# An expert's third tile of rows turned only where it has one, rows loaded from GpSimd's queue, and four low parts of the last weights made later

## What is computed

```python
def _moe2_ref(x, w_gate, w1, w2, capacity):
    logits = x @ w_gate                      # x: 1536 rows of 384, E = 8 experts
    expert_idx = np.argmax(logits, axis=1)
    ...                                      # gate_w: the softmax of the chosen one
    for i in range(N):                       # disp[e]: up to capacity = 384 rows
        e = expert_idx[i]
        if counts[e] < capacity:
            disp[e, counts[e]] = x[i]
...
    h = np.maximum(np.einsum('ecd,edf->ecf', disp, w1), 0.0)   # w1[e]: 384 x 1024
    y = np.einsum('ecf,efd->ecd', h, w2)                       # w2[e]: 1024 x 384
    ...                                      # out[i] = gate_w[i] * y[its expert, its place]
```

## Time and profile before

| | |
|---|---|
| median of 3 runs | 420.84 us (420.67 to 420.88) |
| the profiled execution | 420.92 us |
| its span in the trace | 419.2 us (mean granted clock 0.997) |

### The profile page before, as it was taken

The page is one execution under the profiler, slowest core; times in us unless marked ns, Lnnn a source line. Parts: engine busy times, 40 slices in busy tenths (PEclk is TensorE's granted clock), DMA queues, the critical chain, the costliest instruction groups (busy, mean ns, idle before and its releaser), DMA issues.

```text
span 419.2 us, 9352 instructions
## 1 busy us (share of the span) xinstructions
PE 403.1 (96%) x3194; PEld 387.9 (93%) x3195; DVE 265.4 (63%) x571; ACT 191.4 (46%) x442; POOL 183.6 (44%) x191
## 2 busy tenths in 40 slices
PE   5799999999999999999999999999999999999992
PEld 5698899999999999999999999998999999999972
DVE  6898877664427434264333789582888797735990
ACT  2879955341221212211123333343859595626950
POOL 3999808554222442224435567253503031103252
PEclk9999999999999999999999999999999999999998
DMA  6997027436980000000100245316996694908500
GB/s 236 405 380 248 3 65 215 148 101 230 367 301 0 35 24 0 0 0 19 38 0 0 75 132 155 111 42 223 378 360 176 211 291 142 322 5 258 165 3 27
DMA packets 34329, 61.74 MB, mean 147 GB/s; under 512 B 4798, under 2 KB 27310, under 8 KB 34288
## 3 DMA queue, kind: packets, MB, share of 16 engines
q1 hardware_dynamic: 31280, 55.92, 39.7%
q0 software_dynamic: 3008, 5.29, 3.7%
HBM read 47.92 MB, written 15.18 MB: 151 GB/s over the span
## 4 chain that ended last, share of the span: by engine, by line
PE 86%; DVE 5%; issue 2%; POOL 2%; PEld 1%; ACT 1%; DMA 0%; POOLq 0%; DVEq 0%; PEldq 0%; ACTq 0%
PE bank L1436 24%; PE bank L1397 23%; PE bank L1619 8%; PE bank L1650 5%; PE bank L1670 4%; PE bank L1720 3%; PE bank L1381 3%; PE bank L1345 2%; PE bank L1373 2%; PE bank L1685 2%; PE bank L1537 2%; PE bank L1588 1%; PE bank L1331 1%; PE bank L1547 1%; PE bank L1445 1%
## 5 line engine op out<-in xcount | busy, mean ns | idle before, releaser
L553 POOL TENSOR_TENSOR g_low<-act_full,g_high 128x384 fp32r<-128x384 f32 x63 | 65.1, 1034 | 111.3 <-ACT g_high L697 111.2
L697 ACT ACTIVATE g_high<-act_full 128x384 fp32r<-128x384 f32 x64 | 33.7, 526 | 146.1 <-DVE act_full L1032 133.5
L1397 PE MATMUL bank<-x_split,w_high 128*128 (+1 forms) x384 | 98.6, 337 | 0.2 <-DVE w_low L945 0.2
L1026 DVE TENSOR_SCALAR neg<-bank,alpha_sb 128x384 f32<-128x384 f32 x64 | 39.4, 616 | 89.0 <-PE bank L1397 89.0
L1397 PEld LDWEIGHTS bank<-x_split,w_high 128*128 128x128 f32 x384 | 68.9, 188 | 0.9 <-DVE w_low L945 0.5
L611 POOL DMA_INDIRECT out<-y_out,token x24 | 30.9, 1289 | 86.2 <-ACT y_out L823 83.0
L1436 PE MATMUL bank<-w_high,g_high 128*128 128x384 f32 x189 | 64.5, 341 | 0.0
L1397 PE MATMUL bank<-x_split,w_low 128*128 (+1 forms) x192 | 64.4, 336 | 0.0
L1436 PE MATMUL bank<-w_high,g_low 128*128 128x384 f32 x189 | 63.8, 338 | 0.0
L1436 PE MATMUL bank<-w_low,g_high 128*128 128x384 f32 x189 | 63.8, 338 | 0.0
L1032 DVE SCALAR_TENSOR_TENSOR act_full<-bank,neg 128x384 f32<-128x384 f32 x64 | 35.7, 557 | 2.4
(11 more groups left out here) (171 smaller groups left out, 841.9 us busy)
## 6 DMA issues: line engine op xcount, KB each, us to landing
w_raw<-chunks SPq DMA_DIRECT2D x96, 192.0 KB, 5.9
w_raw<-chunks SPq DMA_DIRECT2D x32, 384.0 KB, 3.8
rk_in<-att_rk SPq DMA_DIRECT2D x12, 704.0 KB, 6.5
routed_rows<-fill SPq DMA_DIRECT2D x1, 5211.0 KB, 18.0
xe<-routed_rows SPq DMA_DIRECT2D x7, 579.0 KB, 5.4
v_in<-att_v SPq DMA_DIRECT2D x12, 200.0 KB, 6.3
out<-fill SPq DMA_DIRECT2D x1, 2304.0 KB, 23.3
x_split<-x_split POOLq DMA_DIRECT2D x18, 48.0 KB, 2.6
```

The source lines that it names most:

```text
L553: pool.tensor_tensor(gl[:, f % 4, :], act_full[:, f % 2, :], gh[:, f % 4, :].bitcast(f32), ALU.subtract).then_inc(s_gl, 1)
L697: act.activation(gh[:, f % 4, :], act_full[:, f % 2, :], ACT.Copy).then_inc(s_gh, 1)
L1026: dve.tensor_scalar(neg[:, f % 2, :], h, 0.0, alpha_sb[:, f:f + 1], ALU.min, ALU.mult)\
L1397: last = mm(bank[f % 4][:, 0:G], a[:, f, w], x[:, kc, bass.ds(g * G, G)], start=kc == 0 and i == 0, stop=kc == KC - 1 and i == 2)
```

## The change

1. The third tile of an expert's rows is no longer turned during the expert before. It is turned at the head of the expert's own three-tile side, with ACT's and DVE's split there too; the products f = 0 and 1 of tile 0's `expert_down` are moved from behind `flip_up(e, 2, ...)` to between the turn and it. New semaphores count these third tiles; experts without one only raise them.
2. The rows of experts 2 to 7 are loaded from GpSimd's queue. `load_xe(e + 2)` stands before expert e's three scatters, behind the wait for the scatters of e - 1, and waits until expert e's third tile is turned (or passed over). SP's queue holds only the weights.
3. Expert 7's low parts of `w2` for f = 4 to 7 move from expert 6's one-tile side into expert 7's, between its `flip_relu` and `flip_low`.

```diff
         def xe_there(engine, e, tiles):
 
-            if e:
-                engine.wait_ge(s_xe[e % 2], (e + 1) // 2 * 16)
+            if e >= 2:
+                engine.wait_ge(s_xep[e % 2], e // 2 * 16)
+            elif e:
+                engine.wait_ge(s_xe, 16)
...
-        TURN = {3: 0, 5: 1, 7: 2}
+        TURN = {3: 0, 5: 1}
...
             def load_xe(e):
-                if e >= 2:
-                    sp.wait_ge(s_te, (e - 2) * GT + 1 if e > 2 else 2)
-                    sp.wait_ge(s_meta, e - 1)
-                elif e:
+                if e:
...
                 for f in range(NFE):
                     load_w1(e, f)
-                load_xe(e)
                 for f in range(NFE):
                     load_w2(e, f)
...
+            def load_xe(e):
+
+                pool.wait_ge(s_te2 if e > 2 else s_te, e - 2 if e > 2 else 2)
+                pool.wait_ge(s_meta, e - 1)
+                pool.dma_start(xe[:, e % 2, :, :],
+                               disp[ER + e * CAP:ER + (e + 1) * CAP, :].rearrange("(i p) n -> p i n", p=P))\
+                    .then_inc(s_xep[e % 2], 16)
+
...
                 for i in Y_ORDER:
+                    if i == Y_ORDER[0] and e + 2 < E:
+                        load_xe(e + 2)
                     y_scatter(e, i, s_out if e < E - 1 else s_last)
...
-            for i in range(1, GT):
-                xe_high(1, i, bank[X_BANK[i]])
+            xe_high(1, 1, bank[X_BANK[1]])
...
+                    xe_high(e, 2, bank[X_BANK[2]])
                     flip_high(e, 2)
...
+                    def last_low2(*fs):
+                        for f in fs:
+                            if e == E - 1:
+                                split_low2(E - 1, f)
+
                     flip_relu(e, 0, 0)
...
+                    last_low2(4, 5)
                     flip_relu(e, 0, 1)
                     last_low1(3)
+                    last_low2(6)
                     flip_low(e, 0, 0)
+                    last_low2(7)
...
                     if e < E - 1:
-                        for i in range(1, GT):
-                            xe_low(e + 1, i, bank[X_BANK[i]])
+                        xe_low(e + 1, 1, bank[X_BANK[1]])
+                    dve.sem_inc(s_tel2, 1)
                     last_low1(6, 7)
                     if e == E - 2:
-                        low2(0)
-                    low2(1, 2, 3, 4, 5, 6, 7)
+                        low2(0, 1, 2, 3)
+                    else:
+                        low2(1, 2, 3, 4, 5, 6, 7)
...
+                    xe_low(e, 2, bank[X_BANK[2]])
                     for half in range(2):
                         flip_relu(e, 2, half)
...
                 elif i:
-                    pe.wait_ge(s_tel, (e - 1) * GT + GT + 1)
+                    pe.wait_ge(s_tel2, e)
...
                     if more(e):
-                        for i in range(GT):
+                        for i in range(2):
                             x_bank_free(e, i)
                             turn_xe(e + 1, i, bank[X_BANK[i]], 1 - b)
...
                     no_tile(2)
+                    pe.sem_inc(s_te2, 1)
...
                 with pe.Else():
+                    turn_xe(e, 2, bank[X_BANK[2]], b)
+                    expert_down(e, 0, b, range(2))
                     for half in range(2):
                         flip_up(e, 2, half, b)
                     pe.sem_inc(s_w1free, 1)
-                    expert_down(e, 0, b, range(HF))
+                    expert_down(e, 0, b, range(2, HF))
                     flip_turn(e, 2)
```

More of the change, by code:

```diff
@@ L189, in attention_moe_kernel @@
         s_xe0 = [sem(f"first_xe_tile_loaded{i}") for i in range(GT)]
-        s_xe = [sem(f"xe_loaded{i}") for i in range(2)]
+        s_xe = sem("expert_1_rows_loaded")
+        s_xep = [sem(f"expert_rows_loaded{i}") for i in range(2)]
         s_out = sem("out_scattered")
@@ L801, in xe_high @@
             def xe_high(e, i, src):
-                if e:
-                    act.wait_ge(s_te, (e - 1) * GT + i + 2)
+                if not e:
+                    act.wait_ge(s_te0 if i else s_te, max(i, 1))
+                elif i == 2:
+                    act.wait_ge(s_te2, e)
                 else:
-                    act.wait_ge(s_te0 if i else s_te, max(i, 1))
+                    act.wait_ge(s_te, (e - 1) * 2 + i + 2)
                 act.activation(xeh[:, e % 2, :, i * P:(i + 1) * P],
-                               src[:, 0:DM].rearrange("p (k n) -> p k n", k=KC), ACT.Copy).then_inc(s_teh if e or not i else s_teh0, 1)
+                               src[:, 0:DM].rearrange("p (k n) -> p k n", k=KC), ACT.Copy)\
+                   .then_inc((s_teh2 if i == 2 else s_teh) if e else s_teh0 if i else s_teh, 1)
             def y_copy(e, i):
@@ L880, in _ @@
                     if e < E - 1:
-                        for i in range(1, GT):
-                            xe_high(e + 1, i, bank[X_BANK[i]])
+                        xe_high(e + 1, 1, bank[X_BANK[1]])
+                    act.sem_inc(s_teh2, 1)
                     if FIRST <= e + 1 < E:
@@ L1167, in xe_low @@
             def xe_low(e, i, src):
-                if e:
-                    dve.wait_ge(s_teh, (e - 1) * GT + i + 2)
+                if not e:
+                    dve.wait_ge(s_teh0 if i else s_teh, max(i, 1))
+                elif i == 2:
+                    dve.wait_ge(s_teh2, e)
                 else:
-                    dve.wait_ge(s_teh0 if i else s_teh, max(i, 1))
+                    dve.wait_ge(s_teh, (e - 1) * 2 + i + 2)
                 place_ = (slice(0, P), e % 2, slice(0, KC), slice(i * P, (i + 1) * P))
                 dve.tensor_tensor(xel[place_], src[:, 0:DM].rearrange("p (k n) -> p k n", k=KC),
-                                  xeh[place_].bitcast(f32), ALU.subtract).then_inc(s_tel if e or not i else s_tel0, 1)
+                                  xeh[place_].bitcast(f32), ALU.subtract)\
+                   .then_inc((s_tel2 if i == 2 else s_tel) if e else s_tel0 if i else s_tel, 1)
             def keep_meta(e):
@@ L1242, in _ @@
             flip_low(0, 0, 1)
-            for i in range(1, GT):
-                xe_low(1, i, bank[X_BANK[i]])
+            xe_low(1, 1, bank[X_BANK[1]])
             for c in range(2 * NF - 3, 2 * NF):
@@ L1291, in _ @@
                             xe_low(e + 1, TURN[f], bank[X_BANK[TURN[f]]])
-                        if FIRST <= e + 1 < E:
+                        if FIRST <= e + 1 < E and not (e == E - 2 and f >= HF):
                             split_low2(e + 1, f)
+                        if e == E - 1 and f < HF:
+                            split_low2(e, HF + f)
                     if e == E - 2:
@@ L1582, in turn_xe @@
                     pe.wait_ge(s_xe0[i], 16)
-                elif b:
-                    pe.wait_ge(s_xe[1], (e + 1) * 8)
+                elif not isinstance(e, int) or e > 1:
+                    pe.wait_ge(s_xep[b], (e - b) * 8)
                 else:
-                    pe.wait_ge(s_xe[0], e * 8)
+                    pe.wait_ge(s_xe, 16)
                 for kc in range(KC):
                     last = pe.transpose(dst[:, kc * P:(kc + 1) * P], xe[:, b, i, kc * P:(kc + 1) * P], ident[:, :])
-                last.then_inc(s_te if later(e) or not i else s_te0, 1)
+                last.then_inc((s_te2 if i == 2 else s_te) if later(e) else s_te0 if i else s_te, 1)
             def flip_banks_free(e, b):
@@ L1598, in x_bank_free @@
             def x_bank_free(e, i):
-                if i < 2:
-                    y_bank_free(e, GT - 1 - i)
-                else:
-                    pe.wait_ge(s_tel, (e - 1) * GT + GT + 1)
+                y_bank_free(e, GT - 1 - i)
             def y_bank_free(e, i):
```

15 lines of the change are left out of this document (7 added, 8 removed).

## The result

The changed kernel takes **421.66 us** in the median (420.74 to 422.68), the kernel before 420.9 (420.67 to 421.97). The ratio is 1.0015, with a 95% interval from 1.0009 to 1.0021: about 0.6 us slower, where 2 us faster was predicted. The profiled execution took 422.55 us with a span of 420.7, so it is one of the slower ones.

A forecast was written before the change was run, and what follows sets the result against it. PE, busy 96% of the span, was taken to bound the kernel except at the end. Turns -1.98, third-tile wait +0.3, end -1.1 and expert 2's rows +0.7 gave -2.1 from 420.84: 418.8 us, range 417.7 to 421.0.

The forecast's parts named there:

- turns and third tile: Part 1 on PE: six turns fewer, -1.98 us, against a new wait at expert 4's third tile, +0.3.
- The turns: Six third-tile turns of 0.33 us each leave PE's list, each counting in full: -1.98 us.
- so the full 0.33 counts there: One-tile sides, between `flip_turn` halves: PE would still arrive 0.2 us behind the second `flip_relu`, so each turn saves 0.33.
- The third tile's wait: Expert 4, between third tile's turn and its up: PE waits about 0.3 us; bounds nothing to 1.38.
- the whole 1.71 of expert 0: Expert 0's turn-to-first-matmul time, taken for expert 4; less 1.39 of turn and six products, 0.32 us wait.
- The end: Expert 7, last up matmul to first down product: gap falls from 2.64 to 1.55 us, saving 1.1; bounds 0 to 1.3.
- half a turn 0.36: Last term of the 1.55 us gap at expert 7's end, taken from expert 5 (386.14 to 386.50).
- Expert 2's load: On GpSimd from 297.31, taking 7.2 us, needed at 303.8: PE waits 0.7 us.
- Expert 7's load: On GpSimd behind expert 4's last scatter: there at about 392, needed at 393.9, so no wait.
- Rival (b): DVE's `w_low` shuts GpSimd out, expert 2's load 3.5 to 6.3 us late: 421.6 to 424.4 us; chance 0.09.

The follow-up runs named there:

- e3: The changed kernel with expert 2's load one step earlier on GpSimd, ahead of its last `w_low`: 420.01 us, ratio 0.9970.
- e6: The kernel before with only the third tiles' turns moved, row loads on SP's queue: 420.42 us, ratio 0.9983.
- e5: The kernel before with only the four `w_low` of expert 7 moved behind its first `flip_relu`: 420.16 us, ratio 0.9975.
- e17: e8 with the loads of experts 2, 4 and 6 on SP's queue, three left on GpSimd: 419.22 us, ratio 0.9965.
- e18: e8 with each of the six GpSimd loads issued as three, one per tile (eighteen transfers): 421.37 us, ratio 1.0011.
- e11: e3 with the second tile turned twice in the sides of experts 1 to 4: 421.21 us, ratio 1.0011.
- e7: e3 with the second tile turned twice in the three one-tile sides (experts 0, 5, 6): 420.59 us, ratio 0.9989.
- e8: e3 with nine down products instead of six ahead of the third tile's up: 419.64 us, ratio 0.9968.
- e2: The changed kernel with the row loads on SP's queue, expert 2's in its old place: 420.11 us, ratio 0.9961.
- e9: e2 with expert 2's load behind its second weights in SP's list: 421.30 us, ratio 1.0011.
- e13: The changed kernel unaltered, one profiled execution: 421.63 us.
- e16: e3 unaltered, one profiled execution as a control: 420.93 us.
- e1: The changed kernel measured again, unaltered: 421.38 us, ratio 1.0004.
- e4: The kernel before with only the loads of experts 2 to 7 moved to GpSimd's queue: 423.18 us, ratio 1.0038.
- e10: The changed kernel with SP holding expert 2's second weights until expert 2's rows have landed: 421.63 us, ratio 1.0014.

## Why the prediction was wrong

It gave 418.8 us and 421.66 were measured, outside the range. (The range's lower end, 417.7, comes to 417.9 by its own terms, which changes nothing.) The sum against what the runs showed, in us:

| term | predicted | measured | from |
|---|---|---|---|
| turns and third tile | -1.68 | -0.62 | e3, e6 at expert 6 |
| end (part 3) | -1.1 | -1.0 | e3, e5 |
| expert 2's rows | +0.7 | +1.16 | five profiles against e3 |
| GpSimd's closing | 0 | +0.48 | e17, e18 |
| start | 0 | +0.71 | five profiles, cause open |
| sum | -2.1 | +0.73 | medians: +0.76 |

- **The turns, -1.98.** Three of the six stood in two-tile sides and count in full (0.32 each by e11). The other three stood in one-tile sides and bring 0.25 together by the profiles of e7 and e3 (by the times 0.6 to 0.8). The step that failed is "so the full 0.33 counts there": the prediction looked at `flip_relu` of the second half alone and not at ACT's `flip_high` of the first, for which the down products wait next. In expert 5 that takes half of a turn; where the rest goes is open. 0.74 us.
- **The third tile's wait, +0.3.** The wait on `xe_low` is 0.29 as forecast, but PE loses more around it. In its timeline the up starts 1.84 us after the turn (368.44 to 370.28) for work of 1.38, which is 0.46 lost (e8: 1.91 with three products of 0.176 more, no wait), and the up itself takes 4.22 us, against 4.11 in e8. The prediction took the whole 1.71 of expert 0 as the way from turn to up. Covering the whole (e8) brought 0.57. 0.27 us.
- **The end, -1.1.** Right in size: 1.05 in the time of e5, 0.86 to 1.04 in the profiles. The gap itself closed to 1.76 us and not to 1.55, in the changed kernel and in e5. The term "half a turn 0.36" was too small: 0.58 (407.89 to 408.47; 406.07 to 406.65 in e5), again with the first down product 0.21 us after the end of ACT's first `flip_high`. It is the same oversight as with the turns.
- **Expert 2's load, +0.7.** Right in mechanism and place, too small. It was to start at 297.31 and take 7.2; it started at 297.11 to 298.40, later where the whole was later, and took 6.95 to 8.45. The Trainium skill's formula ("DMA: Bandwidth & Descriptors", section "Anatomy of one DMA"), which gave 3.4 us, held for none of these loads; with the engines freed it took 4.3.
- **Expert 7's load.** Right: started at 390.51, landed 5.2 us later, some 1.6 us before PE turned the rows. From SP's list, at 389.98 and 390.33, it was late (e2, e9).
- **Rival (b)**, GpSimd shut out by DVE: wrong for the load itself, which took 0.82 us at 298.40. The sharper test is expert 7's load: issued at 390.51, beside seven `w_low` on DVE from 390.41 for 3.36 us, it took 0.79.
- **Not in the prediction at all:** 0.08 us at the program's end for each load moved to GpSimd. The prediction counted what the loads hold up and not what they leave behind.

**Open** is the start. The first dense matmul stands at 55.88 to 56.04 in the profiles of the five kernels with all loads on SP, and between 55.87 and 57.20 in the fourteen profiles of kernels with loads on GpSimd beside e17's 55.90. The code ahead of it is the same. Whether the changed program stops there more often, or five and fourteen executions fell so, was not settled; the 0.71 us are the mean of five profiles of the changed kernel, and a single profile of the kernel before stands against them. The sum is built from these profiles, so that it comes out at the medians' difference says only that together they are typical of the kernel, not that each term is. Two times speak against a start that belongs to the change. e3's profiled 420.90 us hold 1.02 us of late start, and its median is 420.01, its fastest execution 419.84: most of its executions can't have started that late. And the kernel before took 421.78 us in the one execution beside e13 to e16 and had a median of 421.39 beside e1 to e4, so it too has executions 0.5 to 0.9 us above its profiled one; where they lose it was not profiled.

## What to carry to other kernels

Before a load is moved to another queue, ask what stands ahead of it on the new engine and what the transfer engines carry at the new time: here the queue made the load neither faster nor slower, and a start two microseconds earlier was worth 1.4 us (e3 against e1). When work is taken from between two halves of a chain over several engines, follow every branch of the chain to its next consumer; in dense code a matmul taken out counts in full, in a chain it may count for much less (here a quarter by the profiles). Count from a mark just ahead of the changed region when two profiles are compared, since what lies before it can differ by more than the change.

## What was new about the hardware

- Each load of rows that GpSimd issues, of 193 or 579 KB alike, adds 0.08 us to the closing of the program, in the DRAIN of its own queue (7.2, 7.46, 7.7 and 8.67 us after the last `y_copy` for none, three, six and eighteen), long after it has landed.
- The same transfer of 579 KB, issued at nearly the same place, lands after 4.3 us when SP's stream is held and after 7 to 8.6 us beside it, from either queue. The Trainium skill says on "DMA: Bandwidth & Descriptors", section "Queues, rings and completion order", that each engine alternates between the queues that it has work for. By that one would expect GpSimd's load to overtake SP's backlog; at 6.95 to 8.6 us from GpSimd against 7.7 from SP, it did not noticeably do so here.
- The page of the changed kernel counts 864 packets more on GpSimd's queue and 2400 fewer on SP's for the same 3.55 MB: about 4.1 KB a packet against 1.5. The queue's share of the engines' time fell by 2.0 points on SP's and rose by 2.8 on GpSimd's, so in these two profiles larger packets were not cheaper. Before, then after:

```profile
q1 hardware_dynamic: 31280, 55.92, 39.7%
q0 software_dynamic: 3008, 5.29, 3.7%
```

```profile
q1 hardware_dynamic: 28880, 52.37, 37.7%
q0 software_dynamic: 3872, 8.85, 6.5%
```

- A scatter that runs beside DVE's eight `w_low` ends 0.85 us behind them, with full transfer engines (the changed kernel: 301.26 for 3.99 us, against 300.57 for 3.83) and with partly idle ones. In e10, where their share was 0.53 to 0.60 from 300 to 304 us, one took 4.00 us as well:

```profile
300.28 4.00 POOL L613 DMA_INDIRECT out<-y_out,token  x1 [0.30 <-issue]
```

Its end at 304.28 is 0.85 us behind the eight `w_low` of that kernel (from 299.60, 3.83 us), the distance of the earlier trace rows. Why was not tried.
